# Attention and two MLPs on one core: smaller first chunks with whole float32 weights, sixteen weight places and separate stages for the split weights

## The reference, cut to what matters

```python
# attention: q, k, v are (4 batches, 8 heads, 576, 64)
scores = 0.125 * q @ k.T
kth = np.partition(scores, -32, axis=-1)[..., -32:-31]      # 32nd largest of each row
scores = np.where(scores >= kth, scores, -1e9)
attn = softmax(scores)                                       # with 1e-9 added to the sum
x = (attn @ v) laid out as (2304 tokens, 512)
# first MLP, then second MLP
x = (1 / (1 + exp(-(x @ w_gate))) * (x @ w_val)) @ w_out     # 512 -> 1536 -> 512
x = np.maximum(x @ w_in, 0) ** 2 @ w_out2                    # 512 -> 2048 -> 512
```

## Time and profile before

| | us |
|---|---|
| median of 3 runs | 1252.26 (1250.49 to 1252.37) |
| the profiled execution | 1252.19 |
| its span in the profile | 1250.4 |
| PE busy | 1169.2 (94%) |
| DVE busy | 848.4 (68%) |
| ACT busy | 740.7 (59%) |
| POOL busy | 626.3 (50%) |

### The profile page before, as it was taken

The page is one execution under the profiler, slowest core; times in us unless marked ns, Lnnn a source line. Parts: engine busy times, 40 slices in busy tenths (PEclk is TensorE's granted clock), DMA queues, the critical chain, the costliest instruction groups (busy, mean ns, idle before and its releaser), DMA issues.

```text
span 1250.4 us, 21797 instructions
## 1 busy us (share of the span) xinstructions
PE 1169.2 (94%) x7520; PEld 991.9 (79%) x7520; DVE 848.4 (68%) x1756; ACT 740.7 (59%) x1758; POOL 626.3 (50%) x539
## 2 busy tenths in 40 slices
PE   3469989869999999999999999999999999999999
PEld 2248877769999898888888777777778788888999
DVE  7988988737779977788997667688864445610121
ACT  5777778557768756666776666467654443531221
POOL 4875668646648845553664445356543333530220
PEclk9769999989999999999999999999999999999999
DMA  7874667686665785655456555454555545556997
GB/s 262 313 266 143 230 209 225 204 298 225 224 228 199 246 309 192 198 199 170 160 191 230 200 168 191 168 185 153 175 193 194 178 160 181 176 189 212 365 369 263
DMA packets 89245, 270.13 MB, mean 216 GB/s; under 512 B 9904, under 2 KB 15024, under 8 KB 89136
## 3 DMA queue, kind: packets, MB, share of 16 engines
q1 hardware_dynamic: 89136, 268.74, 62.7%
HBM read 228.33 MB, written 40.37 MB: 215 GB/s over the span
## 4 chain that ended last, share of the span: by engine, by line
PE 80%; ACT 6%; POOL 4%; DMA 4%; DVE 4%; issue 2%; SPq 1%; ACTq 0%; DVEq 0%; POOLq 0%
PE ps L497 21%; PE ps L499 19%; PE ps L498 19%; PE ps L438 6%; PE ps L402 5%; PE ps L418 5%; PE ps L483 3%; DMA w_split<-ring 2%; POOL below L728 2%; DVE work L663 2%; DVE top L661 1%; POOL ring L723 1%; ACT scores L529 1%; DMA ring<-w_in 1%; ACT probs L548 1%
## 5 line engine op out<-in xcount | busy, mean ns | idle before, releaser
L728 POOL TENSOR_TENSOR below<-scores,below 128x576 f32<-128x576 f32 x144 | 205.2, 1425 | 297.9 <-ACT below L541 285.5
L661 DVE MAX8 top<-work 128x8 f32<-128x576 f32 x432 | 312.9, 752 | 5.0
L497 PE MATMUL ps<-xy_hi,ring 128*128 128x512 f32 (+3 forms) x800 | 292.1, 365 | 0.3 <-ACT act_buf L597 0.3
L499 PE MATMUL ps<-xy_hi,ring 128*128 128x512 f32 (+3 forms) x800 | 283.2, 354 | 0.0
L498 PE MATMUL ps<-xy_lo,ring 128*128 128x512 f32 (+3 forms) x800 | 283.2, 354 | 0.0
L663 DVE MATCH_REPLACE8 work<-top,work 128x576 f32<-128x576 f32 x288 | 213.8, 742 | 0.0
L497 PE MATMUL ps<-g_hi,ring 128*128 128x512 f32 (+3 forms) x560 | 203.0, 363 | 0.0
L499 PE MATMUL ps<-g_hi,ring 128*128 128x512 f32 (+3 forms) x560 | 197.8, 353 | 0.0
L498 PE MATMUL ps<-g_lo,ring 128*128 128x512 f32 (+3 forms) x560 | 197.6, 353 | 0.0
L497 PEld LDWEIGHTS ps<-xy_hi,ring 128*128 128x128 f32 x800 | 151.4, 189 | 24.8 <-issue 9.7
L687 DVE SCALAR_TENSOR_TENSOR full_buf<-act_buf,ps 128x512 f32<-128x512 f32 (+3 forms) x60 | 35.5, 591 | 193.1 <-PE ps L499 176.7
(11 more groups left out here) (56 smaller groups left out, 1749.9 us busy)
## 6 DMA issues: line engine op xcount, KB each, us to landing
ring<-w_split SPq DMA_DIRECT2D x318, 512.0 KB, 3.7
w_split<-ring SPq DMA_DIRECT2D x68, 512.0 KB, 4.2
ring<-w_in SPq DMA_DIRECT2D x113, 256.0 KB, 3.4
vt<-v_in SPq DMA_DIRECT2D x16, 480.0 KB, 5.3
heads_in<-qk_in SPq DMA_DIRECT2D x16, 336.0 KB, 4.8
vt<-v_in SPq DMA_DIRECT2D x16, 320.0 KB, 4.1
heads_in<-qk_in SPq DMA_DIRECT2D x16, 240.0 KB, 3.8
heads_in<-qk_in SPq DMA_DIRECT2D x8, 368.0 KB, 5.6
```

Of the source, the lines that this page charges most:

```text
L497: nc.tensor.matmul(dst, w_hi, hi[:, k, 0:WIDTH[c]], start=first, stop=False)
L499: mm = nc.tensor.matmul(dst, w_lo, hi[:, k, 0:WIDTH[c]], start=False, stop=final)
L661: nc.vector.max(out=best, in_=sc if step == 0 else wk).then_inc(sel_step[t % 2], 1)
L728: nc.gpsimd.tensor_tensor(out=below[:, t % 2, :], in0=scores[:, t % PLACES, :], in1=below[:, t % 2, :], op=ALU.subtract).then_inc(mask_don ...
```

## The change

CHUNK_BLOCKS becomes (2, 3, 7, 8, 8, 8): widths 128, 192, 448, 512, 512, 512 instead of 192, 384, 448, 512, 512, 256. The first two chunks (NW = 2) use whole float32 weights. While they run, the memory of the ring is 16 places of one whole block each (`wring`), and the split parts go to four stages of their own (`stage`), in memory that `g_lo` uses later; `x1`, the data of chunk 1, lies there too. Loads of whole blocks wait only until PE has used the place's last block and POOL has made its low part; the wait for a store's landing moves to ACT, before it writes a stage again. The store is issued three blocks after its block. Every fourth block is split before the MLPs (NPRE = 17), one fourth in chunk 0, one in chunk 1, and the last fourth five blocks ahead in chunk 2. MLP_AT, worked out by the new constants, is 12, 24, 53, 85, 117, 149; the slots remain 150. `probs_h` gets a second place.

```diff
-CHUNK_BLOCKS = (3, 6, 7, 8, 8, 4)
+CHUNK_BLOCKS = (2, 3, 7, 8, 8, 8)
+NW = 2
...
-RING = 8
+RING, WPLACES, STAGES = 8, 16, 4
 AHEAD = 5
-JOBS = [(None, n, True, True) for n in range(0, NB, 3)]
+STORE_LAG = 3
+CLASSES = NW + 2
+JOBS = [(None, n, True, True) for n in range(0, NB, CLASSES)]
 NPRE = len(JOBS)
-JOBS += [(c, n, c < 2 and c == n % 3 - 1, c == 0 or c == 1 and n % 3 == 2) for c in range(NC) for n in range(NB)]
+JOBS += [(c, n, c + 1 == n % CLASSES, c < NW or c == NW and n % CLASSES == CLASSES - 1)
+         for c in range(NC) for n in range(NB)]
+NWHOLE = NPRE + NW * NB
...
+def jobs_ahead(k):
+    if k < NWHOLE:
+        return [k - WPLACES] if k >= WPLACES else []
+    if k >= NWHOLE + RING:
+        return [k - RING]
+    return [i for i in range(NWHOLE - WPLACES, NWHOLE) if i % WPLACES // 2 == ring_place(k)]
...
-MLP_AT = [CHUNK_END[c] + (6 if c else 5) for c in range(NC)]
+MLP_AT = [CHUNK_END[c] + (5 if c < NW else 6) for c in range(NC)]
...
-        each = 2 * (WIDTH[c] / 0.6 + 6) if c == 0 else 6 * max(WIDTH[c] / 2.33 + 10, 110)
+        each = 2 * (WIDTH[c] / 0.6 + 6) if c < NW else 6 * max(WIDTH[c] / 2.33 + 10, 110)
...
-        probs_h = sb("probs_h", [P, SEQ + B64])
+        probs_h = sb("probs_h", [P, 2, SEQ + B64])
...
         g_hi = sb("g_hi", [P, NJ2, NMAX], F32R)
+        with nc.sbuf_tensor("stage", [P, STAGES, 2, KT * P], F32R) as stage, \
+                nc.sbuf_tensor("x1", [P, NM, NMAX], F32) as x1:
+            pass
         g_lo = sb("g_lo", [P, NJ2, NMAX], F32R)
...
             def load_weights(k):
...
+                for ahead in jobs_ahead(k):
+                    if ahead >= NPRE:
+                        sp.wait_ge(blk_done, ahead - NPRE + 1)
+                    if JOBS[ahead][2] and ahead < NWHOLE:
+                        sp.wait_ge(w_lo_done, SPLIT_OF[ahead] + 1)
+                    elif JOBS[ahead][2]:
+                        wait_stored(sp, ahead)
...
-                    if c == 0 and k in SPLIT_OF:
-                        store_parts(k)
+                    if k - STORE_LAG in STAGE_OF and k - STORE_LAG >= NPRE:
+                        store_parts(k - STORE_LAG)
...
-            for k in range(RING):
+            for k in FIRST_LOADS[:RING]:
                 load_weights(k)
             load_v(1)
+            for k in FIRST_LOADS[RING:]:
+                load_weights(k)
...
             def split_weights(k):
-                act.wait_ge(ring_loaded[k % RING], 16 * (k // RING + 1))
-                nc.scalar.activation(place(k)[:, 0, :], whole(k), ACT.Copy).then_inc(w_hi_done, 1)
+                wait_loaded(act, k)
+                if k < NWHOLE and STAGE_OF[k] >= STAGES:
+                    wait_stored(act, STAGED[STAGE_OF[k] - STAGES])
+                nc.scalar.activation(both_parts(k)[:, 0, :], whole(k), ACT.Copy).then_inc(w_hi_done, 1)
...
                 pool.wait_ge(w_hi_done, SPLIT_OF[k] + 1)
-                if JOBS[k][0] == 0:
-                    pool.wait_ge(blk_done, k - NPRE + 1)
...
+                    if c == NW and j == 0:
+
+                        for k in STAGED[-STAGES:]:
+                            wait_stored(pool, k)
```

More of the change, by code:

```diff
@@ L171 @@
     HEADS_AT.setdefault(max(FIRST_TILE[_g - 1] - 3, 0), []).append(_g)
-for _c in range(1, NC):
+for _c in range(NW, NC):
     for _p in range(PAIRS):
@@ L242, in probs_of, with both_parts @@
             u, part = TILES[t]
-            return probs_h[:, 0:SEQ] if part == 2 else probs[:, RANK[u] % 2, part, :]
-        def place(k):
-            return ring[:, k % RING, :, :]
+            return probs_h[:, RANK[u] % 2, 0:SEQ] if part == 2 else probs[:, RANK[u] % 2, part, :]
         def whole(k):
-            return ring0[:, k % RING, 1, :]
+            return wring[:, k % WPLACES if k < NWHOLE else 2 * ring_place(k) + 1, :]
+        def both_parts(k):
+            return stage[:, STAGE_OF[k] % STAGES, :, :] if k < NWHOLE else ring[:, ring_place(k), :, :]
         const_step = sem("const_step")
@@ L256, in attention_mlps @@
         out_stored = [sem("out_stored0"), sem("out_stored1")]
+        whole_loaded = [sem(f"whole_loaded{i}") for i in range(WPLACES)]
         ring_loaded = [sem(f"ring_loaded{i}") for i in range(RING)]
-        w_stored = [sem(f"w_stored{i}") for i in range(RING)]
+        stage_stored = [sem(f"stage_stored{i}") for i in range(STAGES)]
+        ring_stored = [sem(f"ring_stored{i}") for i in range(RING)]
         w_hi_done = sem("w_hi_done")
@@ L293, in wait, with wait_loaded, wait_stored @@
                 eng.wait_ge(s, count)
[L295 to L301, removed]
+        def wait_loaded(eng, k):
+            if k < NWHOLE:
+                eng.wait_ge(whole_loaded[k % WPLACES], 16 * (k // WPLACES + 1))
+            else:
+                eng.wait_ge(ring_loaded[ring_place(k)], 16 * ring_use(k))
+        def wait_stored(eng, k):
+            if k < NWHOLE:
+                eng.wait_ge(stage_stored[STAGE_OF[k] % STAGES], 16 * (STAGE_OF[k] // STAGES + 1))
+            else:
+                eng.wait_ge(ring_stored[ring_place(k)], 16 * ring_stores(k))
         block = ctx.enter_context(nc.Block())
@@ L343, in mlp_dma @@
                     k = NPRE + c * NB + n
-                    load_weights(k - 1 + RING)
-                    if k + AHEAD in SPLIT_OF and JOBS[k + AHEAD][0] == 1:
+                    for job in LOAD_AT.get(k, []):
+                        load_weights(job)
+                    if k + AHEAD in SPLIT_OF and JOBS[k + AHEAD][0] == NW:
                         store_parts(k + AHEAD)
-                    if c == 0 and k in SPLIT_OF:
-                        store_parts(k)
-                    if kind == "out" and i == parts - 1:
+                    if k - STORE_LAG in STAGE_OF and k - STORE_LAG >= NPRE:
+                        store_parts(k - STORE_LAG)
@@ L351, in mlp_dma @@
+                    if kind == "out" and i == last:
                         sp.wait_ge(out_copied, c * NM + m + 1)
@@ L414, in turn @@
                 half = UNITS[u][4]
-                both = probs_h if half else probs[:, RANK[u] % 2, :, :].rearrange("p h c -> p (h c)")
+                both = probs_h[:, RANK[u] % 2, :] if half else probs[:, RANK[u] % 2, :, :].rearrange("p h c -> p (h c)")
                 for k in range(KFULL + 1 if half else NBLK):
@@ L720, in split_weights @@
                 pool.wait_ge(w_hi_done, SPLIT_OF[k] + 1)
-                if JOBS[k][0] == 0:
-                    pool.wait_ge(blk_done, k - NPRE + 1)
-                nc.gpsimd.tensor_tensor(out=place(k)[:, 1, :], in0=whole(k), in1=place(k)[:, 0, :].bitcast(F32),
+                nc.gpsimd.tensor_tensor(out=both_parts(k)[:, 1, :], in0=whole(k), in1=both_parts(k)[:, 0, :].bitcast(F32),
                                         op=ALU.subtract).then_inc(w_lo_done, 1)
```

132 lines of the change are left out of this document (71 added, 61 removed).

## The result

The changed kernel takes 1243.72 us, median of 7 runs (1240.11 to 1244.82), against 1250.49 for the kernel before in the same comparison (7 runs, 1245.59 to 1252.37). The ratio is 0.9949, interval 0.9928 to 0.9969: 0.5% faster, about 6.8 us, where 32 were forecast. The profiled execution has a span of 1243.0 us and took 1244.82, the longest of the seven. Its mean granted clock is 0.985 of full speed; the shortest, 1240.11, had 0.992.

The account below looks back on a forecast made before the run. PE was taken as the bound, with early losses from DVE's pace and store-load waits. Terms 70.9 + 89 + 154 + 227.8 + 486.9 + 189.1 = 1217.7 us, plus 1.8 gives 1219.5; range 1205 to 1246, 8 times in 10.

Parts of the forecast that it names:

- the sum's ledger: Whole kernel against before: start -24.6, attention +8.7, MLP work +4.6, early chunks' loss -21.5, end +0.7: -32 us.
- transfer rival: Transfers bind the first 160 us; at 292 GB/s chunk 0 ends 22.6 us later, time 1242; chance 0.11.
- lockstep rival: Chunk 0: accumulators and `act_buf` tie PE to ACT and POOL, 116 us instead of 89, time 1246; chance 0.11.
- The slower rival: Chunks 0 and 1: attention step order, not stores, caused the losses; old pace stays, 1264 us; chance 0.06.
- Step 1: Start of the MLPs: in slot 12 instead of 16, first matmul at 70.9 us instead of 95.5.
- Step 2: Chunk 0, 12 slots: 81.7 us of PE work, 4 lost in starting, 3 in jitter; 89 us.
- Step 3: Chunk 1, 29 slots, DVE-bound at 5.35 us: 155, less 3 for DVE's lead, plus 2 entering split form; 154 us.
- The rival of a low clock in chunk 1: A tenth of chunk 1 at 1.2 GHz sets PE 7.7 us back, at worst 1227 us; chance 0.05.
- The lower bound, 145: Chunk 1's shortest expected time in us: DVE floor less its lead.
- Step 4: Chunk 2, 448 wide, 32 slots: old stretch 227.2 us plus 0.6 more attention, 17 splits hidden; 227.8 us.
- Steps 5 and 6: Chunks 3 and 4: 486.9 us with PE full; last chunk: 185.6 us, with the end 3.5.

Follow-up runs that it names:

- e4: The changed kernel's new places and stages with the old widths 192, 384, 448, 512, 512, 256 and only chunk 0 whole: 1233.4 us.
- e3: The kernel before, old weight places kept, with the new widths, splits from slot 0 and the second place of probs_h: 1339.2 us.
- e1: The changed kernel with 4 instead of 16 weight loads ahead of slot 0, the other 12 behind the heads of groups 2 and 3: 1236.8 us.
- e8: From e1, the 17 splits before the MLPs cut to 16 of 512 columns on ACT and POOL; stores stay whole: 1233.0 us.
- e9: From e8, the 34 splits in chunks 0 and 1 cut to 16 of 512 columns too: 1225.7 us.
- e2: The changed kernel with results of chunks 0 and 1 copied to full_buf instead of act_buf: 1239.5 us.
- e5: The changed kernel with both mends, the edits of e1 and e2: 1231.8 us.
- e11: From e5, the 17 splits before the MLPs start in slot 0 instead of slot 2: 1237.4 us.
- e10: From e5, the old widths 192, 384, 448, 512, 512, 256 and only chunk 0 whole: 1232.0 us.

## Why the prediction was right or wrong

**Direction and places: right.** The change is faster, and the old places did stall the kernel: 16.6 us by e4 for places and waits together, where the sum's ledger put 21.5 on the early chunks' losses (its own terms give 41.7 less 20.5, that is 21.2). The time itself, 1243.7, lies inside 1205 to 1246, but by luck: that range reached so far for the transfer and lockstep cases, and neither came. The slower rival (the losses were never the stores') falls by e3 and e4, though part of it is true: e4's slots from 29 to 40 keep 6.1 us.

**Step 1 failed**, and with 11.6 us it is the largest miss. It took slot 12's start over from the old trace and asked only whether ACT would wait for a stage. It did not ask what the eight more loads stand in front of. Each costs SP about 0.48 us (3.84 for 8), and all 16 are 4.2 MB in the 16 DMA engines; the third and fourth groups of heads, whose first tiles are 4 and 6 now and were 6 and 9 before, because groups have two tiles and not three, came behind both. e1 measured 7.6 us of start, 6.9 us of time. The rest, 4.8 us by e8 against e1, is the loop over ACT and POOL that the splits lengthen; in the old rows a lead of scores hid it until slot 9. The sign of it stood there: slots 12 to 15 took 6.2 us where DVE needs 5.2, and yet I wrote that DVE alone set the pace up to the MLPs.
The Trainium skill, Trainium Kernel Development and Optimization, section Key Constraints, says that DMAs from several queues share the same 16 engines, so that issuing from more than one saves only issue time. No run here tried it.

**Step 2 held in its total:** 89.7 us for 89. That its 7 us of losses were a cold start and jitter is not shown: e9 takes only 1.2 us of them away. The lockstep rival (116 us) did not come, nor did the transfer rival: chunk 0 ran at 307 GB/s and a DMA share of 0.85, with PE waiting for no weights. The transfers did bind, but in places that the sum had not asked about: one transfer of heads and one store of results.

**Step 3 failed in two terms.** DVE's lead of a few us, which I took as 3 us of gain, can't be kept: at chunk 1's first val block DVE waits for PE, slot 24 takes 11.7 us even in e2. And the wait of ACT for the stores of chunk 0's results had no term, 4.3 us by e2 with the low clock behind it, 1.7 by e5 against e1 without; it is in the unchanged code, but had cost nothing worth seeing at the old passage. The pace itself, 5.35 a slot, was right: 5.30. The rival of a low clock in chunk 1 came in small: 3.4 of the 161.2 us at 1.2 GHz, not a tenth, and at the passage, not in the stretch that DVE bounds. The lower bound, 145, should have been 143.8 by its own terms (29 x 5.2 less 7).

**Step 4** took chunk 2 from a stretch without splits and named the cover of the splits by the old chunk 1. Its loss against the plan is 9.4 us instead of 4.8. PE waited 4.6 us there for copies of transposes, in three pieces, where it waited 1.5 before; that is 3.1 us of the 4.6. The rest goes with the clock. After the longest of these waits, 2.5 us, the changed kernel's PE ran at 1.2 GHz for 3.4 us:

```profile
PE ps L458 <- ACT pt L618: 4.6, 3, 2.5
...
507.00:510.50 3.50, 1.15 (x12) 0.80 (x14) 3.50 (x9) 3.16 (x9) 3.50 (x3) 1.00 0.01 5
510.50:513.90 3.40, 3.40 (x21) 2.90 (x18) 3.37 (x6) 0.28 (x1) 1.24 (x2) 0.50 0.64 198
```

e1 and e8 have such a piece too, and a chunk 2 of 232.7 and 232.5 us. e2, e5, e9 and e11 have the same waits (4.2 to 4.6 us), no low clock, and 230.7 to 231.2 us. So about 1.4 us go with the clock. Why the waits are longer than before stays open; the 17 splits of this stretch weren't left out in any run.

**Steps 5 and 6 held:** 673.6 and 3.5 us, for 672.5 and 3.5.

**The ledger by cause.** I had the widths as a gain: 24.6 us of start for 8.7 of attention and 4.6 of MLP work. Measured with the new places they cost 10.3, and with both mends nothing (e5 and e10). Even mended, the start gives 19.4 us (93.7 to 74.3); 13.3 are paid for the work that moves, and the rest goes in chunk 1, which DVE bounds (16.0 us over its plan in e5, 6.1 in e10), and in chunk 2.

## What to carry to other kernels

A deeper prefetch at the start of a kernel is not free: count its issues and its bytes ahead of the first transfer that the critical path needs, and put that one first. Before taking a pace from an old trace, ask whether a lead hid a slower loop, and what takes the lead away. A term from unchanged code must be asked for again once its neighbours come closer: here a store's landing between two chunks. And when a wait is priced by taking it away, look at the clock behind it: part of the gain can be the clock's.

## What the runs showed of the hardware

A store of 64 KB of results took 7.2 us to land at 172.7 us, in the middle of 10 us in which the DMA engines moved 409 GB/s; the loads of 256 KB took 4.8 us in the middle, against 3.4 before. One issue on SP took 0.33 us alone (at 77.1 us) and 0.48 in the row of eight at 8.2 us. At 182.8 and 510.5 us in the changed kernel and at 81.7 us in e1, PE had a granted clock of 0.50 for 3.4 us, soon after waits of 3.0, 2.5 and 2.7 us; after the same wait of 2.5 us in chunk 2, e2 kept 1.00. The stretch in which the store landed:

```profile
170.00:180.00 10.00, 8.62 (x63) 7.92 (x61) 3.69 (x11) 5.90 (x14) 5.94 (x5) 1.00 1.05 409
```
